# A fused attention and mixture-of-experts kernel: the first pair's k from a second queue, part of the router's weights between the first score groups, and one batch's choice a pair later

## The reference

```
scores = scale * q @ k.T        (causal mask, softmax) ; local = a @ v
mem_out = (phi(q) @ M_prev) / (phi(q) @ z_prev + 1e-6) ; phi(x) = max(x,0) + min(exp(x),1)
x = g * mem_out + (1 - g) * local          g = sigmoid(beta)
```

```
logits = x @ w_gate ; e = argmax(logits) ; gate = softmax(logits)[e]
out = gate * sigmoid(x @ w_output_gate)[e] * (relu(x @ w1[e]) @ w2[e])
```

## Time and profile before

| | |
|---|---|
| median of 3 runs | 474.15 us (474.09 to 474.35) |
| profiled execution, its own time | 473.32 us |
| its span, first to last instruction | 471.2 us |
| mean granted TensorE clock | 0.996 of full |
| PE busy / PEld busy | 454.6 us (96%) / 357.9 us (76%) |
| DVE / ACT / POOL busy | 304.5 / 278.2 / 187.7 us |

### The profile page before, as it was taken

How to read it: one execution, slowest core, us unless ns; L and a number is a source line. 1 busy time by engine, 2 the same in 40 slices (tenths; PEclk the granted TensorE clock), 3 DMA queues, 4 the chain that set the end, 5 groups by cost and what they waited for, 6 DMA issues and landing times.

```text
span 471.2 us, 11873 instructions
## 1 busy us (share of the span) xinstructions
PE 454.6 (96%) x4252; PEld 357.9 (76%) x4253; DVE 304.5 (65%) x799; ACT 278.2 (59%) x623; POOL 187.7 (40%) x182
## 2 busy tenths in 40 slices
PE   8999999999999999999999989999999899899994
PEld 6677777776777768788888878888888688788873
DVE  4788798899989998876222688222247948942220
ACT  6888888899999875445222675222257637732220
POOL 7567776679897645251222111211112111011111
PEclk9999999999999999999999999999999999999998
DMA  7244433567544803557222389200118947300000
GB/s 231 78 116 141 125 102 104 181 204 218 191 112 136 270 28 102 200 177 293 69 67 68 112 291 317 91 27 23 45 52 294 326 157 266 118 2 22 22 24 36
DMA packets 44880, 64.04 MB, mean 136 GB/s; under 512 B 7198, under 2 KB 26142, under 8 KB 44832
## 3 DMA queue, kind: packets, MB, share of 16 engines
q1 hardware_dynamic: 40672, 53.81, 35.1%
q0 software_dynamic: 4160, 9.60, 6.4%
HBM read 56.77 MB, written 10.90 MB: 144 GB/s over the span
## 4 chain that ended last, share of the span: by engine, by line
PE 91%; DVE 4%; issue 4%; ACT 0%; POOL 0%; ACTq 0%; DVEq 0%; POOLq 0%
PE S L1454 20%; PE S L1631 19%; PE S L1632 18%; PE S L1633 18%; PE STK L1454 4%; PE TP_ps L1454 4%; DVE probs L955 3%; PE TP_ps L1671 2%; PE STK L1666 2%; PE TP_ps L1450 2%; PE STK L1450 2%; DVE neg_max L955 1%; PE TP_ps L1654 0%; PE S L1643 0%; POOL out L682 0%
## 5 line engine op out<-in xcount | busy, mean ns | idle before, releaser
L734 ACT ACTIVATE probs<-probs,neg_max 128x128 f32<-128x128 f32 (+2 forms) x144 | 82.9, 581 | 8.8 <-DVE neg_max L955 8.4
L682 POOL DMA_INDIRECT out<-x_ring,slot_tok_i x23 | 24.1, 1048 | 147.7 <-ACT x_ring L819 125.0
L1631 PE MATMUL S<-w_hi,x_hi 128*128 128x512 f32 x180 | 70.2, 390 | 0.0
L1633 PE MATMUL S<-w_hi,x_lo 128*128 128x512 f32 x180 | 70.1, 389 | 0.0
L1632 PE MATMUL S<-w_lo,x_hi 128*128 128x512 f32 x180 | 70.0, 389 | 0.0
L607 POOL DMA_INDIRECT x_ring<-x_tokens,slot_tok_i x29 | 33.1, 1140 | 80.7 <-DMA out<-x_ring,slot_tok_i 63.1
L1454 PE MATMUL S<-k_pair,q_pair 64*128 64x256 f32 (+5 forms) x384 | 62.9, 441 | 0.0
L1631 PE MATMUL S<-w_hi0b,hid_hi 128*128 128x512 f32 x152 | 61.7, 406 | 0.0
L955 DVE CUSTOM_DVE_ANT_0 probs<-S,mask 128x128 f32<-128x128 f32 (+3 forms) x128 | 55.1, 486 | 7.9 <-PE S L1454 7.2
L1632 PE MATMUL S<-w_lo0b,hid_hi 128*128 128x512 f32 x152 | 59.4, 391 | 0.0
L1633 PE MATMUL S<-w_hi0b,hid_lo 128*128 128x512 f32 x152 | 59.2, 389 | 0.0
(11 more groups left out here) (232 smaller groups left out, 862.8 us busy)
## 6 DMA issues: line engine op xcount, KB each, us to landing
w_raw<-in_moe_w SPq DMA_DIRECT2D x60, 512.0 KB, 5.1
q_pair<-in_qt SPq DMA_DIRECT2D x15, 288.0 KB, 2.9
k_pair<-in_kt SPq DMA_DIRECT2D x15, 288.0 KB, 3.3
v_nat<-in_v SPq DMA_DIRECT2D x16, 256.0 KB, 3.6
x_tokens<-x_out SPq DMA_DIRECT2D x16, 256.0 KB, 2.4
x_ring<-in_moe_w SPq DMA_DIRECT2D x2, 512.0 KB, 4.9
m_aug<-in_m_aug SPq DMA_DIRECT2D x1, 648.0 KB, 6.2
m_turned<-in_m_t SPq DMA_DIRECT2D x1, 512.0 KB, 3.8
```

What stands on the lines that cost most here:

```text
L682: nc.gpsimd.indirect_dma_start(out=out[:, :], out_offset=bass.IndirectOffsetOnAxis(ap=slot_tok_i[:, t:t + 1], axis=0), in_=x_ring[:, t % X ...
L734: last = nc.scalar.activation(pr, pr, ACT.Exp, bias=neg_max[:, slot, h:h + 1], scale=-1.0, accum_out=sums[g % 2][:, at, 0:1])
L1631: T.matmul(dst, hi, part(i, k)[:, cols], start=first, stop=False)
L1633: return T.matmul(dst, lo, part(i, k)[:, cols], start=False, stop=last)
```

## The change

It has three parts.

1. **Loads.** ACT issues k first, k rest, w_pair and betas, ahead of its own first work, and SP no longer does. SP loads m_turned in two DMAs, pairs 0 to 5 and pairs 6 to 15 (`MW_PARTS`), with a semaphore for each.
2. **Router's weights.** `router_weights` is cut into two calls. The first, for 6 pairs (12 matmuls), stands behind `scores(0, 0)` in place of the three matmuls of zeros; the second, for 10 pairs (20 matmuls), stands where the whole stood, and no longer waits for `masked` 6, since the result now goes to `STK`. `turn(0, 3)`, which writes `STK` too, waits for `mw_copied` in return. DVE's `memory_weights` moves from the end of step 0 to the place ahead of `mask_row(0, 7)`. Of the five matmuls of zeros at the start four are left.
3. **Batch 1's choice.** `choose(1)` moves from step 9 (behind) to step 10 (ahead), `so_far(1, 2)` from step 10 to 12, `rank(1)` on PE from pair 10 to 11, `read_ranks(1)` and `place(1)` from step 10 to 11, `lanes(0)` from step 11 to 10.

```diff
             load_qk(0)
-            sp.dma_start(betas[:, :], beta.rearrange("(a h) -> a h", a=1).broadcast_to([P, H])).then_inc(ld_beta, 16)
-            sp.dma_start(w_pair[:, :, :], w_pair_in).then_inc(ld_mt, 16)
-            sp.dma_start(m_turned[:, :, :], m_t_in).then_inc(ld_mt, 16)
+            for n, part in enumerate(MW_PARTS):
+                sp.dma_start(m_turned[:, part, :], m_t_in[:, part, :]).then_inc(ld_mt[n], 16)
...
+            act.dma_start(k_pair[0][:, 0:2 * P], kt[0, 0, :, 0:2 * P]).then_inc(ld_first, 16)
+            act.dma_start(k_pair[0][:, 2 * P:S], kt[0, 0, :, 2 * P:S]).then_inc(ld_qk[0], 16)
+            act.dma_start(w_pair[:, :, :], w_pair_in).then_inc(ld_wp, 16)
+            act.dma_start(betas[:, :], beta.rearrange("(a h) -> a h", a=1).broadcast_to([P, H])).then_inc(ld_beta, 16)
             act.wait_ge(ld_beta, 16)
...
                     routing_ahead(g)
+                    if g == 0:
+                        memory_weights()
                     mask_row(g, 7)
...
-                if g == 0:
-                    memory_weights()
...
                 elif k == 3:
+                    if l == 0:
+                        pe.wait_ge(mw_copied, 1)
...
-            def router_weights():
-                pe.wait_ge(ld_mt, 32)
-                pe.wait_ge(masked, 6)
-                for t in range(G):
+            def router_weights(n):
+                pe.wait_ge(ld_wp, 16)
+                pe.wait_ge(ld_mt[n], 16)
+                for t in range(G)[MW_PARTS[n]]:
...
-            zero_products(5)
+            zero_products(4)
...
                 if g == 0:
-                    zero_products(3)
+                    router_weights(0)
...
-                    router_weights()
+                    router_weights(1)
...
-    RANK_PAIR = {7: 0, 10: 1, 14: 2}
+    RANK_PAIR = {7: 0, 11: 1, 14: 2}
```

More of the change, by code:

```diff
@@ L67, in memory_attention_top1_moe @@
     TLW = TL + 2
+    MW_PARTS = (slice(0, 6), slice(6, G))
     assert VOID >= N and EARLY_TILES < FAR and N < FAR * P
@@ L228, in memory_attention_top1_moe @@
     ld_beta = sem("ld_beta")
-    ld_mt = sem("ld_mt")
+    ld_wp = sem("ld_wp")
+    ld_mt = [sem(f"ld_mt{n}") for n in range(2)]
     ld_maug = sem("ld_maug")
@@ L430, in memory_attention_top1_moe @@
     LATE_SLOTS = STK[:, 1, 0:2 * (ES - EARLY_TILES)]
-    RANK_PAIR = {7: 0, 10: 1, 14: 2}
-    READS = {6: 1, 7: 2, 10: 3, 14: 4}
+    RANK_PAIR = {7: 0, 11: 1, 14: 2}
+    READS = {6: 1, 7: 2, 11: 3, 14: 4}
     with ctx, nc.Block(no_gpsimd_drain=True) as block:
@@ L452, in load_qk @@
                     sp.dma_start(q_pair[u][:, 0:2 * P], qt[b, p, :, 0:2 * P]).then_inc(ld_first, 16)
-                    sp.dma_start(k_pair[u][:, 0:2 * P], kt[b, p, :, 0:2 * P]).then_inc(ld_first, 16)
                 sp.dma_start(q_pair[u][:, rest], qt[b, p, :, rest]).then_inc(ld_qk[u], 16)
-                sp.dma_start(k_pair[u][:, rest], kt[b, p, :, rest]).then_inc(ld_qk[u], 16)
+                if g > 0:
+                    sp.dma_start(k_pair[u][:, rest], kt[b, p, :, rest]).then_inc(ld_qk[u], 16)
             def load_v(g):
@@ L903, in memory_weights @@
                 dve.wait_ge(mw_done, 1)
-                V.tensor_copy(m_aug[:, :, D:HC], O_ps[:, P:P + G * RE].rearrange("r (g e) -> r g e", e=RE)).then_inc(mw_copied, 1)
+                V.tensor_copy(m_aug[:, :, D:HC], STK[:, 0, 0:G * RE].rearrange("r (g e) -> r g e", e=RE)).then_inc(mw_copied, 1)
             def turning_weights():
                 dve.wait_ge(consts, 3)
-                dve.wait_ge(ld_mt, 32)
+                dve.wait_ge(ld_wp, 16)
                 dve.wait_ge(consts_dve, 3)
@@ L1102, in read_ranks @@
                     sel.then_inc(rank_read, 1)
-                    dve.wait_ge(rank_read, READS[(7, 10)[b]])
+                    dve.wait_ge(rank_read, READS[(7, 11)[b]])
                 else:
@@ L1190, in routing_ahead @@
                 elif g == 10:
+                    choose(1)
                     open_gate(1)
-                    so_far(1, 2)
                 elif g == 11:
                     scale(1)
+                elif g == 12:
+                    so_far(1, 2)
                 elif g == 13:
@@ L1217, in routing_behind @@
                     largest(1)
-                    choose(1)
                 elif g == 10:
+                    lanes(0)
+                elif g == 11:
                     read_ranks(1)
                     place(1)
-                elif g == 11:
-                    lanes(0)
                 elif g == 12:
@@ L1515, in local @@
                 last.then_inc(loc_mm, 1)
-            def router_weights():
-                pe.wait_ge(ld_mt, 32)
-                pe.wait_ge(masked, 6)
-                for t in range(G):
+            def router_weights(n):
+                pe.wait_ge(ld_wp, 16)
+                pe.wait_ge(ld_mt[n], 16)
+                for t in range(G)[MW_PARTS[n]]:
                     for h in range(2):
                         half = slice(h * D, (h + 1) * D)
-                        last = mm(O_ps[half, P + t * RE:P + (t + 1) * RE], m_turned[half, t, :], w_pair[half, t % NPAIR, :], True, True)
-                last.then_inc(mw_done, 1)
+                        last = mm(STK[half, 0, t * RE:(t + 1) * RE], m_turned[half, t, :], w_pair[half, t % NPAIR, :], True, True)
+                if n == 1:
+                    last.then_inc(mw_done, 1)
             def count_first():
```

## The result

The changed kernel takes 476.07 us (median of 22 runs, 474.14 to 478.43), the kernel before 474.57 us beside it. The ratio is 1.003, 95% interval 1.0016 to 1.0044: the change costs 1.5 us, where -1.89 us was forecast. The profiled execution takes 476.52 us with a span of 474.8 us, against 473.32 and 471.2. One of the 22 runs of the kernel before took 744.66 us and does not enter the ratio.

A forecast was written before the change was run, and what follows sets the result against it. PE, busy for 96% of the span, was taken as the bound. First pair -1.24 us and batch 1's choice -0.65 us sum to -1.89 us, from 474.15 to 472.3 us; range 471.6 to 474.2 us.

The forecast's parts named there:

- Scores start 0.2 us earlier: Start of first pair: k issued by ACT lands at 3.2 us, scores 0.2 us earlier (0 to 0.45), worth nothing by itself.
- So ACT is not late.: Loads: betas, ACT's fourth issue instead of SP's fifth, land about 0.5 us earlier, ahead of the first scores' masks.
- m_turned's first part by 5.3: First pair: data for the router's first part lands at 5.3 us (3.9 to 5.5); second score group starts 0.15 us earlier.
- The clock up about 7 us: First pair: PE's weight loads for scores at 187 ns from about 7 us; no term of its own in the sum.
- The second part, -0.70: First pair, ahead of the tail: 40 router records take 1.16 us against 1.86 for the whole, -0.70 us.
- no masked wait, -0.13: First pair: router's second part follows the transposes at 9.46 us without waiting for `masked` 6, -0.13 us (0 to 0.15).
- The copy to m_aug ahead of the tail's mask, -0.26: First pair: DVE's copy fits idle time, memory product waits for ACT's copy, starts at 14.70 against 14.96, -0.26 us.
- Part 3, -0.65: Step 10: without `choose(1)` ahead of unit 3's copy, the memory product follows the local product, -0.65 us (-0.2 to -0.86).
- (a): First pair: PE's clock rises some 3 us later, +1.3 us, total -0.6, 473.6 us; chance 0.20.
- (b): PE's clock stays low through the first pair, not risen by about 10.5 us: total +1.9, 476.0 us; chance 0.08.
- (c): m_turned's first part lands near 6.2 to 6.5, second score group at about 7.6: total -0.9, 473.3 us; chance 0.10.
- The baseline: Whole kernel: median of the runs shown, 0.83 us above the profiled execution's 473.32, taken as starting point, 474.15 us.

The follow-up runs named there:

- e4_nochoice: Changed kernel with batch 1's choice put back as in the kernel before: 476.01 us, 1.0052 of the kernel before.
- e12_spearly: Changed kernel with all loads issued by SP, betas and w_pair right behind the first q and k: 476.93 us, 1.0051 of the kernel before.
- e3_nozeros: Kernel before without its three matmuls of zeros behind the first scores: 475.86 us, 1.0034 of the kernel before.
- e18_fitfill: Changed kernel, all loads on SP with early betas and w_pair, six matmuls of zeros at the start, five ahead of the router's first part: 473.15 us, 0.9978.
- e6_best: Kernel before with batch 1's choice moved, router's weights whole to STK without the masked wait, memory_weights ahead of the tail's mask: 474.39 us, 0.9984.
- e13_fill: As e6_best, but six and four matmuls of zeros instead of five and three: 472.86 us, 0.9973 of the kernel before; repeated, 472.79 us, 0.9973.
- e1_choice: Kernel before with only the moves of batch 1's choice: 473.14 us, 0.9975 of the kernel before.
- e10_sparse: Kernel before with the three matmuls of zeros behind the first scores replaced by 14 small ones on zeros: 476.71 us, 1.0037 of the kernel before.
- e11_kact: Kernel before with only k of pair 0 issued by ACT, betas and w_pair staying on SP: 474.48 us, 1.0007 of the kernel before.
- e2_loads: Kernel before with only the changed loads (k, w_pair, betas on ACT; m_turned in two DMAs): 477.88 us, 1.0068 of the kernel before.
- e8_zeros: Changed kernel with three matmuls of zeros ahead of the router's first part: 475.15 us, 1.0006 of the kernel before.
- e16_earlyfill: Changed kernel, all loads on SP with early betas and w_pair, six matmuls of zeros at the start, nine ahead of the router's first part: 474.94 us, 1.0014.
- e14_zeros64: Kernel before with six and four matmuls of zeros instead of five and three, nothing else: 474.51 us, 1.0013 of the kernel before.

## Why the prediction failed, step by step

The forecast was -1.89 us and the medians moved +1.50; 476.07 lies above the upper end of the range, 474.2. In the profiles the first pair is off by 3.45 us (+2.21 against -1.24), and the rest of what was forecast came. Two steps failed, each enough in the traces to lose the first pair's gain: the sum let the loads land in time (betas without a price, m_turned's first part at 5.3), and it let the clock rise about 7 us although it took away the zeros.

- **Scores start 0.2 us earlier.** Wrong: k took 2.9 us instead of 2.2 and landed at 3.7, outside the ends of 3.0 and 3.45. It cost nothing by itself, but it opened a 0.65 us gap among the zeros.
- **"So ACT is not late."** Wrong. I compared places in the issue order (fourth against fifth) and took the landing time as given. Betas landed 5.9 us after their issue, at 8.1, and raised the estimated floor of the first pair to 20.05 us, 1.25 above the 18.80 of before. In e4_nochoice, the same first pair, this was the chain (20.38). I had priced k and m_turned from rows, but for w_pair and betas, which moved as well, I had no row and gave no bounds. The trace of before has them: 3.0 and 2.6 us, on SP.
- **m_turned's first part by 5.3.** Wrong: it landed at 6.8, and w_pair, which this step also needs, at 7.02. This is what the profile's chain starts with. All on one queue m_turned came at 6.78 (e12_spearly). My upper end of 5.5 was too low on either queue. The first part's cost, 1.3 us, was right (1.46).
- **The clock up about 7 us.** Wrong, and only a rival had it. The sum gave the second score group its 1.90 us of before. It took 3.36, because the clock rose at 13.2 us. Without the zeros it rises at 11.1 us also in the kernel before (e3_nozeros), and with seven zeros more the loss of e12_spearly is gone (e18_fitfill).
- **The second part, -0.70, and no masked wait, -0.13.** Right in size where the clock is high: e18_fitfill has 1.18 us from the second part to the tail against 1.86. In the changed kernel it was 1.56.
- **The copy to m_aug ahead of the tail's mask, -0.26.** Right. It costs nothing, and the memory product waits for ACT's copy, as forecast, in the changed kernel, e6_best, e13_fill and e18_fitfill. With the router's whole move it was worth 0.54, against 0.39 for these two terms in the sum.
- **Part 3, -0.65.** Right: 0.67 in the changed kernel and 0.66 in e1_choice, with no part of it given back.
- **The rivals.** (a), (b) and (c) were each partly true at once: m_turned late (c, with 8.46 where 7.6 was named), and the clock up at 13.2 us, past (a) and past the 10.5 us from which (b) decides. (b)'s time, 476.0, came out nearly to the number, but not by its sum: the tail's scores (1.17 us) and the memory product (1.35) ran at the high level, the loads were late, and no rival had the betas' floor (1.25 us up). That the number fits is luck. The error of the chances was to take them as alternatives. They are tied to each other: a late load makes the gap, and the gap and the small matmuls stand where the zeros had held the clock. (a)'s doubt was answered by e10_sparse: the small matmuls did not bring the clock's rise. With 0.38 for the three as separate cases, the forecast kept 0.50 and the slower side had 0.11.
- **The baseline.** The sum was taken from one profile of before, whose first pair had an early clock. That profile was 0.83 us under the median, which I added as a constant; e1_choice shows that such a difference can sit in the first pair, the very stretch that was changed.

## What to carry to other kernels

Filler work at the start of a kernel may be holding TensorE's clock: before it is replaced by useful work, ask whether that work holds the clock as the filler does (small matmuls did not, e10_sparse) and whether its data is there at that time; if not, keep the filler until the data lands (e18_fitfill against e12_spearly, 3.8 us), and no longer. When loads move to another engine, price every one of them, the few KB ones above all, and follow who waits for each; here 4 KB of betas held ACT and POOL and set the first pair's floor. Don't take one profile for the kernel where a load can land early or late: look at the same stretch in a second execution. Waits that grow out of each other are one case, not several with a chance each.

## What the runs showed of the hardware

- **Matmuls of 64 x 16 leave the clock low although TensorE is busy.** With 1.68 us of them behind the first scores the clock was up at 10.3 us (e10_sparse), with nothing there at 11.1 (e3_nozeros, where PE also waited for k), with 128 x 128 matmuls there at 7.0, at 9.2 and 9.4 when PE had also waited 0.39 and 0.25 us for a load (e1_choice, e11_kact), but at 5.0 in e2_loads with a wait of 0.22. These are single executions; the medians of the first two, 1.0037 and 1.0034 of before, bear them out. With full matmuls unbroken from 1.11 us to the second score group it was up at about 7 us in two profiles (before and e6_best, five matmuls of zeros at the start) and at 4 to 6 us in the six profiles with six matmuls of zeros there (e13_fill to e18_fitfill).
- **The clock can fall soon after it rose.** In e2_loads it was up at 5.0 us and down again at 11.8, behind idle stretches of 0.20, 0.77 and 0.65 us and during the router's small matmuls; in e11_kact up at 9.4 and down at 12.8, behind 0.47 us of idle and the same small matmuls. Near 370 us a wait of 1.66 to 1.85 us is sometimes followed by a drop for about 3 us that costs 1.5, and sometimes not, in one and the same program.
- **Small loads on the second queue are slow.** w_pair and betas took 5.3 and 5.9 us behind k on ACT's queue (4.6 and 5.8 in e2_loads, 6.3 and 6.7 in e8_zeros); on SP's queue, right behind the first q and k, they took 2.5 and 2.8 (e16_earlyfill). Which of the two, the second queue or what stood ahead of it and beside it, makes the difference was not separated. The Trainium skill, "DMA: Bandwidth & Descriptors", section on why small descriptors are slow, puts the overhead on a row of 256 bytes, w_pair's length, at 27%. These rows show w_pair taking twice as long on ACT's queue as on SP's, with rows of the same length.
- **A wait of 0.6 to 0.7 us of ACT near 180 us**, at `180.74` in the chain after, stands in every profile except that of the kernel before, also where ACT's program is unchanged (e14_zeros64). What releases it the trace doesn't say, and it stays open. That the profiled execution of before was lucky by that much is likely, but there is only one profile of it.
